# The second token pair's x split over units five to seven instead of five to eight, in a fused attention and two-layer feed-forward kernel

## The reference

```python
scores = (1.0 / S) * np.matmul(z, z.transpose(0, 2, 1))      # z: 2 x 3008 x 64
x = u * np.matmul(np.maximum(scores, 0.0) ** 2, v)           # u, v: 2 x 3008 x 256
x = x.reshape(6016, 256)
h = x @ w_in                                                 # 256 x 2048
x = (h - np.tanh(h)) @ w_out                                 # 2048 x 256
gate = 1.0 / (1.0 + np.exp(-(x @ w_gate)))                   # 256 x 1536
out = (gate * (x @ w_val)) @ w_out2                          # 1536 x 256
```

## Time and profile before

| | |
|---|---|
| median of 3 runs | 1505.71 us (1503.69 to 1505.8) |
| the profiled execution, its own time | 1505.03 us |
| span of the profiled execution, first to last instruction | 1503.2 us |
| mean granted TensorE clock | 0.998 |
| TensorE busy | 1493.6 us, 99% of the span |
| VectorE busy | 1134.4 us, 75% |
| ScalarE busy | 948.8 us, 63% |

### The profile page before, as it was taken

One profiled execution on the slowest core, in us unless ns is written; L12 is line 12 of the kernel. 1 busy time (PEld: TensorE's weight loads), 2 busy tenths in 40 slices (PEclk: granted clock), 3 DMA queues, 4 the chain that ended last, 5 costly groups with the idle time before them and its releaser, 6 DMA issues.

```text
span 1503.2 us, 21910 instructions
## 1 busy us (share of the span) xinstructions
PE 1493.6 (99%) x8808; PEld 1292.2 (86%) x8808; DVE 1134.4 (75%) x1413; ACT 948.8 (63%) x1284; POOL 0.5 (0%) x5
## 2 busy tenths in 40 slices
PE   9999999999999999999999999999999999999998
PEld 8999999888888878888888889888888888888898
DVE  8999988999988776767776777676666676666655
ACT  7777667777766665666666666655555555555654
POOL 0000000000000000000000000000000000000000
PEclk9999999999999999999999999999999999999999
DMA  4443422245433445454535446553635454454352
GB/s 133 145 157 133 156 98 80 96 175 193 159 120 143 156 147 179 146 181 153 208 121 202 155 152 236 192 186 129 244 127 213 158 197 174 190 182 186 134 209 88
DMA packets 36325, 241.79 MB, mean 161 GB/s; under 512 B 3584, under 2 KB 6656, under 8 KB 22912
## 3 DMA queue, kind: packets, MB, share of 16 engines
q1 hardware_dynamic: 36080, 240.17, 43.7%
q10 hardware_dynamic: 144, 0.23, 0.0%
HBM read 196.21 MB, written 44.17 MB: 160 GB/s over the span
## 4 chain that ended last, share of the span: by engine, by line
PE 97%; DVE 1%; ACT 0%; issue 0%; DMA 0%; SPq 0%; DVEq 0%
PE acc L492 25%; PE hidden L456 12%; PE hidden L458 12%; PE hidden L457 12%; PE acc L456 10%; PE acc L457 10%; PE acc L458 10%; PE hidden L479 6%; DVE part_lo L920 0%; DVE h L994 0%; DMA snap<-zT 0%; DVE region L920 0%; DVE h L1041 0%; ACT snap L759 0%; DVE h L1033 0%
## 5 line engine op out<-in xcount | busy, mean ns | idle before, releaser
L920 DVE TENSOR_TENSOR part_lo<-h,part_hi 128x1024 fp32r<-128x1024 f32 (+3 forms) x317 | 375.0, 1183 | 78.7 <-ACT part_hi L767 49.7
L759 ACT ACTIVATE snap<-hidden 128x512 f32<-128x512 f32 (+1 forms) x360 | 211.5, 588 | 254.4 <-PE hidden L458 254.1
L456 PE MATMUL hidden<-region 128*128 128x512 f32 (+1 forms) x840 | 324.9, 387 | 2.0 <-issue 1.9
L457 PE MATMUL hidden<-region 128*128 128x512 f32 (+1 forms) x840 | 324.4, 386 | 0.0
L458 PE MATMUL hidden<-region 128*128 128x512 f32 (+1 forms) x840 | 324.3, 386 | 0.0
L492 PE MATMUL acc<-part_hi,region 64*128 64x512 f32 (+1 forms) x2256 | 288.6, 382 | 0.7 <-ACT part_hi L817 0.7
L994 DVE TENSOR_TENSOR h<-hidden,snap 128x512 f32<-128x512 f32 (+1 forms) x252 | 170.7, 677 | 147.8 <-ACT snap L759 119.1
L456 PE MATMUL acc<-part_hi,region 128*128 128x512 f32 (+1 forms) x672 | 259.2, 386 | 0.3 <-DVE part_lo L920 0.3
L457 PE MATMUL acc<-part_lo,region 128*128 128x512 f32 (+1 forms) x672 | 259.0, 385 | 0.0
L458 PE MATMUL acc<-part_hi,region 128*128 128x512 f32 (+1 forms) x672 | 258.9, 385 | 0.0
L492 PEld LDWEIGHTS acc<-part_hi,region 64*128 64x128 f32 x2256 | 234.5, 184 | 19.9 <-DVE region L920 1.1
(11 more groups left out here) (62 smaller groups left out, 1157.5 us busy)
## 6 DMA issues: line engine op xcount, KB each, us to landing
region<-ready SPq DMA_DIRECT2D x33, 2304.0 KB, 8.8
region<-ready SPq DMA_DIRECT2D x51, 1408.0 KB, 6.0
ready<-region SPq DMA_DIRECT2D x6, 2304.0 KB, 7.6
ready<-region SPq DMA_DIRECT2D x8, 1408.0 KB, 6.1
xs<-x_out SPq DMA_DIRECT2D x20, 512.0 KB, 4.9
x_in<-xs SPq DMA_DIRECT2D x20, 512.0 KB, 7.8
snap<-vP SPq DMA_DIRECT2D x24, 256.0 KB, 2.7
u_in<-uT SPq DMA_DIRECT2D x10, 512.0 KB, 5.4
```

Of the source, the lines that this page charges most:

```text
L456: pe.matmul(dst, w_hi, x_hi, start=start, stop=False, skip_group_check=True)
L457: pe.matmul(dst, w_hi, x_lo, start=False, stop=False, skip_group_check=True)
L759: act.activation(snap[:, g % 2, i, 0:w], hidden[:, CHAIN[g % 2], 0:w], ACT.Copy).then_inc(s_snap, 1)
L920: return ve.tensor_tensor(dst, whole, hi.bitcast(F32), ALU.subtract)
```

## The change

`x_splits` gets a case for pair 1. Slots 0 and 1 stay in unit 4 of pair 0. Slot 4 moves from unit 6 to unit 5, so that unit 5 splits three slots (2, 3, 4). Slot 6 moves from unit 7 to unit 6, which splits 5 and 6. Unit 7 splits none. The same holds for ScalarE's and VectorE's lists. The other pairs and the sums are as they were, and no instruction is added or removed.

```diff
 def x_splits(q, u):
-    u -= q == 1
+    if q == 1:
+        return {4: (0, 1), 5: (2, 3, 4), 6: (5, 6)}.get(u, ())
     return (2 * u - 6, 2 * u - 5) if 3 <= u < 6 else (6,) if u == 6 else ()
```

## The result

| | before | changed |
|---|---|---|
| median of 18 runs each | 1504.68 us (1503.48 to 1506.38) | 1502.16 us (1501.33 to 1502.8) |
| ratio | | 0.9983, 95% interval 0.9977 to 0.9989 |
| span of the profiled execution | 1503.2 us | 1501.0 us |
| mean granted clock in it | 0.998 | 1.000 |

The changed kernel is 2.5 us faster, 0.17%. The forecast time, 1502.1 us, was met, but in part by luck: the gain is 2.5 and not 3.58 us, and the three runs that it started from had a median of 1505.71 where 18 have 1504.68. Two errors of one us cancelled.

The account below looks back on a forecast made before the run. TensorE was taken to bound the kernel, 97% of a 1503.2 us span. Stall -2.09, clock -1.72 and third slot +0.23 made -3.58 us, from 1505.71 to 1502.1 us; range 1500.6 to 1504.5.

Parts of the forecast that it names:

- The wait called "issue": TensorE's wait before unit 8: released by VectorE's split of slot 6; moving it to unit 6 saves 2.09 us.
- The rival that the change does not do what it says: Before unit 8: something other than VectorE's split ends the wait, the stall stays, 0.23 us added, 1505.9 us; chance 0.05.
- Nothing else is late at the start of unit 8: Start of unit 8: weights there 4.0 us early, snapshots and sums as at n = 16, so no wait remains.
- SyncE's queue at no cost: Pair 2's x loads follow unit 9's weights sooner, at about 559.8 us; unit 9 does not wait, cost 0.
- The rival on the other side: Pair 2's x loads hold up unit 9's weights; slower once landing takes 13.6 us, say 1509.1 us at 17; chance 0.04.
- The third slot, 0.23 us: Third split in unit 5 delays ScalarE's first snapshot of unit 6, making TensorE 0.23 us late at product six.
- The clock, -1.72 us: Unit 8: with the gap gone nothing lowers TensorE's clock, so the unit's extra 1.72 us are saved.
- the first rival: Clock in unit 8: its fall need not happen every execution, or moves to unit 6; gain 1.86 us, 1503.85; chance 0.19.

Follow-up runs that it names:

- slot 4 alone: Against the changed kernel, slot 6 goes back to unit 7, so only slot 4's move to unit 5 remains; 1505.29 us, ratio 1.0 to before.
- slot 6 alone: Against the changed kernel, slot 4 goes back to unit 6, which splits 4, 5 and 6; 1501.86 us, ratio 0.998 to before.
- four slots: Against the changed kernel, slot 5 also moves to unit 5, which splits 2, 3, 4, 5, and unit 6 only slot 6; 1502.29 us, ratio 0.9984.
- slot 6 in the idle time: Against before, slot 6 is split in the middle of unit 7, where ScalarE and VectorE idle, not at its end; 1501.84 us, ratio 0.9983; again 1501.81 us.

## Why the prediction was right, and where it was not

*The wait called "issue" is slot 6.* Right, and no longer an inference from two engines starting together: the gap follows the last split, 1.49, 2.09, 2.69 and 3.30 us when it ends 0.60 us earlier, as before, and one and two splits later, and is gone when slot 6 is done in unit 6 or in mid-unit 7, whichever way the other slots lie. The rival that the change does not do what it says falls with it.

*Nothing else is late at the start of unit 8.* Right: units 7 and 8 at 10.2 us after.

*SyncE's queue at no cost.* Right: the same order and 0.42 us as at n = 16, and unit 9 on time. The rival on the other side did not come (its 13.6 us would have been 2.3 times the median of 6.0, not twice).

*The third slot, 0.23 us.* Measured 0.27 in the first profile and 0.26 in three more (10.46 us, with slot 4 alone and in the changed kernel's second and third profile); with slot 6 alone, in unit 7, it was 0.28. The model behind it, snapshot's end plus 0.39 us, gave the 0.78 of four slots. The clock did not fall behind either of these delays.

*The clock, -1.72 us.* Here the step failed, as a term that was mis-sized: a fall costs about what was said, but it does not come in every execution. The sum took it whole, since the one trace had it. Of the 1.72 us some 0.10 comes behind any gap, fall or not, so the fall itself is about 1.62 (1.44 to 1.75 between the groups' means). In the runs of before it is there about half the time (18 of 33, 15 of 33, 13 of 27), and a mean over runs gets about half of it: 2.09 + 0.10 - 0.26 + 0.5 x 1.62 = 2.74 us against 2.56 between the means of the 18 runs each (1504.79 and 1502.23). That was the first rival's mechanism, to which it gave 0.19; its form was too coarse, since it had the median of before either with the fall or without, where the coin lands nearly even and the median of before can sit between two groups. From three runs of which two were in the upper group the prediction took 1505.71 as its base; that rival's 1503.85 is 1.86 us, the gain without a fall, below this same 1505.71, though a time in the upper group has the fall in it. The Trainium skill (TensorE: Matmul & The Clock Gate, Part 1: The HAM clock gate) says that the clock's monitor runs free of the kernel, so that the number of slow matmuls at a kernel's start differs from run to run. Carried over to a fall in mid-kernel, by that rule a single trace can't tell how often a fall comes; the runs agree, with 46 of 93 of before in the upper group.

What is shown of that: two groups 1.44 to 1.75 us apart in before and one group in kernels with no gap or a gap of 1.49 us; traces of a 2.09 us gap with a fall (two kernels, both executions with a mean clock of 0.998) and of 2.69 and 3.30 us gaps without one, both in the lower; and mean clocks of 1.0 in lower groups only and of 0.998 in upper groups only. What was not had: a trace of before itself without the fall. Why the fall comes in one execution and not in the next is open.

## What to carry to other kernels

A wait that the profile gives no releaser is found by looking which other engine goes at the same instant on the same semaphore. Before moving work away from a wait, look for idle time inside the units and not only for a lighter unit: at a unit's end a third split held up a snapshot that had 0.26 us of slack, in the middle it was free. And a fall of TensorE's clock in one profile is one draw: its price goes into a forecast times the share of runs that show it, which the list of run times gives once it is sorted and looked at for groups, with the mean clock of each run beside it.

## What the runs showed of the hardware that was not expected

First, stalls of 2.69 and 3.30 us left the clock at 2.4 GHz in some executions, while one of 2.09 us was followed by some 3.5 us at 1.2 GHz in others. The fall did not begin in the gap but behind it: in before work resumed at 561.29 us and the matmuls were at half pace from about 562.3 on, 1.0 us later; with slot 4 alone it resumed at 562.14 and the clock was still full in 562 to 563, with a mean of 0.77 in 563 to 564, so it fell some 1.3 us later. A stall without a fall costs 0.08 to 0.13 us beyond its length (unit 8 at 10.28, 10.29 and 10.33 us).

Second, the executions scatter by 0.8 to 1.7 us (once 2.3) even without any fall, and part of that arises in attention. In the tiles of 448 columns a step takes either 3.04 or 3.10 us. ScalarE's Relu in the last tile, before:

```profile
454.20 0.90 ACT L823 ACTIVATE h<-hidden 128x896 f32<-128x896 f32 x1
457.24 0.90 ACT L823 ACTIVATE h<-hidden 128x896 f32<-128x896 f32 x1
460.28 0.90 ACT L823 ACTIVATE h<-hidden 128x896 f32<-128x896 f32 x1
```

And after:

```profile
454.92 0.91 ACT L824 ACTIVATE h<-hidden 128x896 f32<-128x896 f32 x1
458.02 0.90 ACT L824 ACTIVATE h<-hidden 128x896 f32<-128x896 f32 x1
461.12 0.90 ACT L824 ACTIVATE h<-hidden 128x896 f32<-128x896 f32 x1
```

TensorE has no wait there in either, and the granted clock is 1.00 in both; its matmuls of this shape have a median of 362 ns before and 365 ns after, from 448 to 480 us (shortest, median and longest behind the colon):

```profile
L492 PE MATMUL acc<-part_hi,region x176: 358/362/366, 447.8 to 479.8; 64*128 64x448 f32 x176
```

```profile
L493 PE MATMUL acc<-part_hi,region x174: 358/365/366, 448.2 to 479.8; 64*128 64x448 f32 x174
```

The two narrow tiles, the last of each batch, give about 1.0 of the 1.30 us by which the changed kernel's profiled execution was behind when the first layer began (483.03 against 481.73 us). The instructions are the same in both kernels. Of two later profiles, the one of slot 4 moved alone had the slower step in the last tile only (457.27 to 475.87 us in six steps) and the one of slot 6 moved alone in neither. The slowest run of a kernel without a gap, 1503.32 us with slot 6 in the idle time, was profiled too: it has the slower step in both tiles and the full clock throughout, so its time is no fall. What sets the pace is open; no experiment here went into it.
